# A pad tile taken out and three index tiles moved in the SBUF layout of an attention, expert and feed-forward kernel

## What is computed

```python
def _attn_ref(x, state):                # x [8, 8, 512, 64], state [8, 8, 32, 64]
    scores = scale * np.matmul(x, state.transpose(0, 1, 3, 2))
    a = softmax(scores)
    xread = np.matmul(a, state)
    scores2 = scale * np.matmul(state, x.transpose(0, 1, 3, 2))
    sread = np.matmul(softmax(scores2), x)
    return np.concatenate([xread, sread], axis=2)

def _moe_ref(x, expert_emb, tau, w1, w2):          # 8 experts, 512 -> 1024 -> 512
    expert_idx = np.argmax(logits, axis=1)
    for e in range(E):
        mask = expert_idx == e
        h = np.maximum(x[mask] @ w1[e], 0.0)
        out[mask] = gate_w[mask, None] * (h @ w2[e])

def _moe2_ref(x, w_in, w_out, s, b):               # 512 -> 2048 -> 512
    r = np.maximum(x @ w_in, 0.0)
    return (s * (r * r) + b) @ w_out
```

## The kernel before

| tile | starts at byte | past a multiple of 64 | past a multiple of 256 |
|---|---|---|---|
| `w_in_hi` | 20512 | 32 | 32 |
| `w_raw` | 86048 | 32 | 32 |
| `x_a`, `w1_hi`, `w_out_hi` | 118816 | 32 | 32 |
| `st_diag` | 163872 | 32 | 32 |
| `x_rows`, `xg`, `y_rows` | 184352 | 32 | 32 |
| `xg_in` | 186400 | 32 | 32 |
| `xg_hi` | 188448 | 32 | 32 |
| `hid_hi` | 196640 | 32 | 32 |
| `y_hi` | 192544 | 32 | 32 |
| `g_hi` | 215072 | 32 | 32 |

## Time and profile before

### The profile page before, as it was taken

How to read it: one execution, slowest core, us unless ns; L and a number is a source line. 1 busy time by engine, 2 the same in 40 slices (tenths; PEclk the granted TensorE clock), 3 DMA queues, 4 the chain that set the end, 5 groups by cost and what they waited for, 6 DMA issues and landing times.

```text
span 1490.1 us, 20856 instructions
## 1 busy us (share of the span) xinstructions
PE 1389.1 (93%) x6774; PEld 1161.8 (78%) x6775; DVE 532.9 (36%) x801; ACT 510.0 (34%) x882; POOL 194.0 (13%) x251
## 2 busy tenths in 40 slices
PE   6999518999999999998699999999999999999998
PEld 5888406888888888886588888888888888888886
DVE  3566681144422144142532242323323232232322
ACT  4677502244433244244232222222222222222221
POOL 1111331222222222222600000000000000000000
PEclk9999758999999999999699999999999999999999
DMA  8677314124442134213110010100101010010000
GB/s 194 195 195 226 108 9 148 42 96 156 151 147 100 42 108 155 81 67 121 43 38 6 0 56 0 56 0 0 56 0 56 0 56 0 0 56 0 29 1 29
DMA packets 88455, 105.22 MB, mean 71 GB/s; under 512 B 44261, under 2 KB 59621, under 8 KB 87920
## 3 DMA queue, kind: packets, MB, share of 16 engines
q1 hardware_dynamic: 82160, 85.52, 18.1%
q0 software_dynamic: 6272, 19.41, 3.7%
HBM read 78.15 MB, written 27.80 MB: 71 GB/s over the span
## 4 chain that ended last, share of the span: by engine, by line
PE 51%; DVE 1%; DVEq 0%; issue 0%; ACT 0%
PE ps_g L1405 25%; PE ps_o L1423 25%; PE ps_yt L1393 1%; DVE w_out_lo L1368 1%; DVE w_raw L1361 0%; DVE g_lo L1351 0%; DVE y_lo L1340 0%; PE ps_o L1441 0%; DVE sq L1348 0%; DVEq L1450 0%; ACT rel L1312 0%; DVEq L1364 0%
## 5 line engine op out<-in xcount | busy, mean ns | idle before, releaser
L1348 DVE TENSOR_TENSOR sq<-rel 128x512 f32<-128x512 f32 (+1 forms) x144 | 96.8, 672 | 493.2 <-ACT rel L1312 493.2
L1312 ACT ACTIVATE rel<-ps_g 128x512 f32<-128x512 f32 (+1 forms) x144 | 82.8, 575 | 534.5 <-PE ps_g L1405 534.5
L1405 PE MATMUL ps_g<-y_hi,w_in_hi 128*128 128x512 f32 (+1 forms) x576 | 219.0, 380 | 3.8 <-DVE y_lo L1340 3.7
L1405 PE MATMUL ps_g<-y_hi,w_in_lo 128*128 128x512 f32 (+1 forms) x576 | 218.4, 379 | 0.0
L1405 PE MATMUL ps_g<-y_lo,w_in_hi 128*128 128x512 f32 (+1 forms) x576 | 218.4, 379 | 0.0
L1423 PE MATMUL ps_o<-w_out_hi,g_hi 128*128 128x512 f32 x544 | 213.5, 392 | 0.2 <-DVE g_lo L1351 0.2
L1423 PE MATMUL ps_o<-w_out_lo,g_hi 128*128 128x512 f32 x544 | 211.9, 390 | 0.0
L1423 PE MATMUL ps_o<-w_out_hi,g_lo 128*128 128x512 f32 x544 | 211.7, 389 | 0.0
L1405 PEld LDWEIGHTS ps_g<-y_hi,w_in_hi 128*128 128x128 f32 x576 | 109.4, 190 | 25.4 <-DVE y_lo L1340 4.1
L1405 PEld LDWEIGHTS ps_g<-y_lo,w_in_hi 128*128 128x128 f32 x576 | 109.4, 190 | 20.6 <-issue 0.2
L1405 PEld LDWEIGHTS ps_g<-y_hi,w_in_lo 128*128 128x128 f32 x576 | 109.4, 190 | 20.0
(11 more groups left out here) (215 smaller groups left out, 1740.5 us busy)
## 6 DMA issues: line engine op xcount, KB each, us to landing
w_raw<-in_moe_w SPq DMA_DIRECT2D x16, 2048.0 KB, 9.7
out_rows<-w_raw SPq DMA_DIRECT2D x34, 256.0 KB, 2.1
x_a<-in_x SPq DMA_DIRECT2D x8, 1024.0 KB, 7.3
x_tok<-x_rows SPq DMA_DIRECT2D x8, 1024.0 KB, 5.3
y_rows<-moe_tok SPq DMA_DIRECT2D x8, 1024.0 KB, 5.6
x_m<-in_x SPq DMA_DIRECT2D x7, 1024.0 KB, 9.4
w_raw<-in_moe_w_out SPq DMA_DIRECT2D x1, 4096.0 KB, 15.1
w_raw<-in_moe_w_in SPq DMA_DIRECT2D x1, 3072.0 KB, 14.0
```

Source lines behind the costliest of these rows:

```text
L1312: nc.scalar.activation(rel[:, k, 0:cols], ps_g[k][:, 0:cols], ACT.Relu).then_inc(rel_ready, 1)
L1348: nc.vector.tensor_tensor(sq[:, 0:cols], rel[:, k, 0:cols], rel[:, k, 0:cols], ALU.mult).then_inc(sq_ready, 1)
L1405: last = nc.tensor.matmul(ps_g[n % 2][:, 0:cols], w[:, wc], a[:, c, 0:cols], start=(c == 0 and w is w_in_hi and a is y_hi), stop=(c == DC ...
```

## The change

`line_pad` is not declared any more. Everything declared after it starts 608 bytes lower (580 rounded up to 32). In the experts' group the three index tiles, of 4 bytes each, are declared behind `xg_in` instead of behind `yg`. They take 32 bytes each, so that `xg_hi`, `xg_lo`, `hid`, `hid_hi`, `hid_lo` and `yg` start 96 bytes higher than without this move. No instruction, wait, DMA or size is changed.

```diff
         tile_tab = sb(top, "tile_tab", [P, 2 * NSLOT + 1], i32)
-        line_pad = sb(top, "line_pad", [P, 145], f32)
         w_in_hi = sb(top, "w_in_hi", [P, DC * F2], f32r)
...
         xg = sb(mo, "xg", [P, D], f32)
         xg_in = sb(mo, "xg_in", [P, D], f32)
+        g_idx0 = sb(mo, "g_idx0", [P, 1], i32)
+        g_idx = sb(mo, "g_idx", [P, 1], i32)
+        s_idx = sb(mo, "s_idx", [P, 1], i32)
         xg_hi = sb(mo, "xg_hi", [P, D], f32r)
         xg_lo = sb(mo, "xg_lo", [P, D], f32r)
         hid = sb(mo, "hid", [P, F], f32)
         hid_hi = sb(mo, "hid_hi", [P, F], f32r)
         hid_lo = sb(mo, "hid_lo", [P, F], f32r)
         yg = sb(mo, "yg", [P, D], f32)
-        g_idx0 = sb(mo, "g_idx0", [P, 1], i32)
-        g_idx = sb(mo, "g_idx", [P, 1], i32)
-        s_idx = sb(mo, "s_idx", [P, 1], i32)
```

## The result

| | median us | runs | ratio to before, 95% interval |
|---|---|---|---|
| before, same comparison | 1490.38 | 1487.78 to 1491.88 | |
| after | 1499.72 | 1499.25 to 1501.81 | 1.0064 [1.0051, 1.0077] |

The change makes the kernel slower by 0.64%, 9.3 us. That is outside 0.2%, so it is not the likeliest case of the prediction (no change, 1490.5). It lies in the range of 1478 to 1512, and it is the size that the rival of slower products gave for the experts alone (1499).

What follows compares the result with a forecast made beforehand. The prediction took the number of PE products times the pace of one to bound the time from about 240 us on; its terms, 0 + 0 + 0 + 0, left the median, 1490.5 us, with a range of 1478 to 1512.

Steps and rivals of the forecast that it cites:

- the likeliest case of the prediction: Whole kernel: no change, 1490.5 us, own range 1487.5 to 1493.5, chance 0.60.
- the rival of slower products: Experts' and feed-forward products start slower, operand pairs in different classes; 4.7 ns each, 1499 us experts alone, 1515 everywhere; 0.13.
- What bounds the kernel, and what a nanosecond is worth: From about 240 us on, time is products times pace; a nanosecond on all 5184 products is 5.2 us, 0.35%.
- PE, later stages: The 5184 fp32r products of experts and feed-forward: new start addresses change their pace by 0, bounds 10.6 ns less, 4.7 more.
- the nearest rows: f32 passes, the only rows with varying address class, were nearest to no difference: classes differ by at most some 5 ns.
- These passes stream at half the rate, so they could hide a cost that fp32r shows: Caveat on using f32 passes, with tolls of 2.9 and 2.5 ns, to bound the fp32r products.
- A start that costs lines along the stream would have grown with the columns: fp32r products: 13.3 ns on top at both 512 and 256 columns, so most misplacement cost is excluded.
- The 13.3 ns: Toll per fp32r product at full clock: 226.7 ns against 213.3 for 512 columns, 120 against 106.7 for 256.
- the price of starting between two lines of 64 bytes: Rival of quicker products: part of the 13.3 ns toll goes; 10.6 ns each, 55 us, 1436 us in full; 0.17.
- The upper bound of 4.7 ns: Most a fp32r product could lose, from the experts' slower earlier steps: 231.4 - 226.7 ns.
- Transfers, DVE and POOL, index tiles: Other address users, each 0: first loads up to 7.3 us slower, routing splits 1 us, index tiles only what they push.
- The forecast's own signs: If right: 12 products in 2.72 us, 246 matmuls per experts' window, 17.5 us attention rounds, 216 and 348 GB/s, 8.3 us wait.

Runs made afterwards that it cites:

- e2: Against the kernel before, only line_pad is taken out, the index tiles stay behind yg; 1489.43 us (before 1489.13), ratio 1.0002.
- e13: Kernel before, feed-forward products reading fixed weight slices, both operands of every second product 32 x n bytes further in block n; 1506.08 us (before 1486.15).

## Why the prediction was wrong

1. *What bounds the kernel, and what a nanosecond is worth*: right. The time is products times pace. The 1824 products of the experts at the measured mean of 5.8 ns more (0.28 us for the 48 of a slot) are 10.6 us.
2. *"PE, later stages", taken as 0*: this is the step that failed. It measured +9.5 us, all of it in the experts. Three things went wrong in it.
   - I asked for the class of a single start (32 or 0 past a multiple of 64). What matters is the distance of the two operands, modulo 256. "Four products with stationary starts at 0, 512, 1024 and 1536 within their tile all run at one pace" was read as proof that starts don't matter; it is a sample of one class only, since all four are multiples of 256. The table of starts that stands ahead of the prediction had the answer: `xg_hi` and `hid_hi` went to 32 past a multiple of 256, all that they are multiplied with to 192.
   - The f32 passes of the earlier trace rows were taken as the nearest rows. They do contain operands at changing distances (the halves of `st_diag` are 1056 bytes apart, the batches 2112, so that all eight multiples of 32 modulo 256 occur), and they show no cost: 222.5 ns a pass in every batch at full clock, before and after. But plain f32 passes don't show this cost (the trace has 16 of them for the 8 matmuls of line 819, at 216 ns for 256 columns, where an fp32r product of 256 takes 120), nor do 256 columns (120 ns), nor half clock (427.5 ns); of what was tried, only fp32r products of 512 columns at the full clock do. The sentence "These passes stream at half the rate, so they could hide a cost that fp32r shows" was the right doubt and should have moved the chance.
   - "A start that costs lines along the stream would have grown with the columns, so most of what misplacement could cost is excluded" fails too. The 13.3 ns were read at distance 0 alone and can't bound what another distance adds; what it adds does depend on the columns, 7 ns at 512 and nothing at 256. The 2.4 columns a nanosecond behind these 13.3 ns can be had from the rows alone: 256 columns more take 226.7 - 120 = 106.7 ns, which is 2.4, and 2 x 120 - 226.7 = 13.3 ns are left over. At half clock (0.50 granted from 718.5 to 730 us before) 213.1 ns for 256 columns are 1.2 a nanosecond, and 427.5 for 512 leave nothing over. That such a toll is partly "the price of starting between two lines of 64 bytes" was my guess, which no run shows: in e2 every large tile starts at 0 past a multiple of 64, and `ps_g` stays at 226.8 ns.
3. *The upper bound of 4.7 ns*: mis-sized. The measured cost is 7.6 ns for `ps_h` and 6.4 for `ps_y` behind the first six steps (7.6 for both behind the first nine, 234.3 for 226.7), 5.8 over the whole slot. The bound came from the slower start of a run of products, which is there in both kernels and says nothing of how dear another distance is.
4. *The rival of slower products*: its mechanism was the right one ("the experts' pair would now stand in different classes"), and its 1499 is what came out, though partly by luck: the price was too low, and the clock's earlier rise gave 1 us back. Its other half, that the feed-forward products change too, did not happen, since both of their operands moved together.
5. *Transfers, DVE and POOL, index tiles, taken as 0*: right, by the rows above. The subtraction of 1024 elements on DVE takes 1220 ns before and after, and 2269 for 2271 beside POOL; "a fixed cost per element" it is not, since 512 elements take 683 to 693 in its subtractions. The index tiles cost only what they push; what they push was the whole effect.
6. *The forecast's own signs*: the chain with 2.72 held and would have misled alone, since it lies in the feed-forward stage. The count in the experts' windows, 241 for 246, was the sign that decided, with "the experts' pace changes alone, if it is the distance between two operands".

That a weight load overlaps the running product does not make it free for that product. In e13, where each product's own operands are a multiple of 256 apart and only the load beside it is off, 226.7 becomes 232 to 237 ns in `ps_o` (230.3 at 192 bytes).

## What to carry to other kernels

Count the distance between the stationary and the moving tile, not the start of either: where fp32r products of 512 columns bound the time, keep tiles that are used together a multiple of 256 bytes apart: here that was 226.7 ns a product against 232 to 234 (28 bytes were as good for one of the two products, and no rule for that was found), and put small tiles at the end of a group, where they push nothing. When a pace seems free of addresses, look which residues the rows really contain before taking that as a zero. A loss of 3% in a product (234.3 ns for 226.7) left the busy share of the experts' windows untouched, 50.00 of 50; the count of instructions in a window (241 for 246) or the step from start to start shows it.

## What was not expected of the hardware

- An fp32r product of 512 columns takes 226.7 ns when its operands are a multiple of 256 bytes apart and 232 to 234 at other multiples of 32; 192 past a multiple is between, 228.3 to 230.7. Between the multiples of 32 it goes from 227.4 (28 bytes, `ps_g`) to 239.5 (20 bytes, `ps_g`), and 4 bytes already cost (232.3, `ps_o`).
- One product at a bad distance slows others: one in three slows all three, and a single shifted load in twelve costs 12 to 24 ns, over two to five products.
- At half clock and at 256 columns the same distance costs nothing that can be seen (427.5 and 120 ns).
